# Expert slots into the dense layer: the last two slots' rows enter the first token block through products, and its gathers start two slots earlier

## Chip, cores and metric

One core of a Trainium2 chip (trn2) runs the whole program. The metric is the device time of one execution in microseconds.

## What is computed

Three layers in a row: attention in which a query sees only keys of its own hash bucket (2 x 8 heads, 768 positions, 64 wide), a mixture of 8 experts with the best two per token, and a dense layer with a rational activation. The change touches the seam between the second and the third:

```python
top2 = np.argpartition(-noisy_logits, 2, axis=1)[:, :2]
...
for e in range(E):
    for k in range(2):
        mask = top2[:, k] == e
        h = np.maximum(x[mask] @ w1[e], 0.0)
        out[mask] += top2_w[mask, k, None] * (h @ w2[e])
# then, with x = out (1536 x 512):
h = x @ w_in
P = a[0] + a[1] * h + a[2] * h2 + a[3] * h3
Q = 1.0 + np.abs(b[0]) * np.abs(h) + np.abs(b[1]) * h2
return (P / (Q + 1e-06)) @ w_out
```

## The kernel before

**Experts.** Tokens are scattered into rows sorted by expert, and these are cut into 31 slots (`SLOTS`) of 128 rows, numbered 0 to 30. TensorE runs, in the call for slot i: `turn_h(i-1)` (8 transposes of the 1024 hidden values, L1128), `up(i)` (24 products with w1, L1110) and `down(i-1)` (24 products with w2 into the bank `ps_o`, L1136). After slot 30's `up` come `turn_h(30)` and `down(30)`. Weights and activations are split into a high and a low part, so every product is three. ScalarE writes the high part of the turned hidden values (L846), VectorE the low part (`split_h`, L1499), and `down` waits for that. VectorE copies a finished slot to `y_sb` (`copy_y`, L1505) and ScalarE's queue stores it to the table `y_slots` in DRAM (`store_y`, L854). In the call for slot i this is the store of slot i-2, issued behind `relu(i)`; the stores of slots 29 and 30 stand behind the loop.

**Seam.** A token's result is the weighted sum of two rows of `y_slots`. The dense layer takes the 1536 tokens in 4 blocks of 384 (`TB` = 3 tiles of 128). For the first block GpSimd waits until all 31 slots are stored (L689, L690) and issues six gathers (L693, two for each tile). ScalarE scales the first row of each token (L888), VectorE adds the second (`combine`, L1528), TensorE turns the sum (`turn_x2`, 4 transposes a tile, L1166), ScalarE and VectorE split it into high and low (L891, L1536), and `product_a` (L1169, 12 products with w_in) can begin.

**Dense layer.** For each of 16 columns of chunks f: `product_a(f)`, a chain of ScalarE, VectorE and GpSimd instructions for the activation (GpSimd's `product`, L704, is one of them), and `product_b(f)` (L1181, 9 products with w_out), which TensorE takes three steps later (`LAG`). `product_a(f)` waits for the activation of f-4.

**GpSimd's order** at the seam is that of its program: the splits of w_in; after `up(30)` two loads of w_out's first half into the high part (`cast_hi`, L577); the six gathers; the loads of the second half; the splits of chunks 0 to 3 of w_out (L569: low part = raw - high; each needs its high part and a raw chunk in a ring of two that SyncE fills when the chunk two before is split, L450); then `product(0, 0)`, then the gathers of the next block (L713) between the products. The second half of that weight buffer is read by `down(30)`, the first half by `up(30)`.

## Time and profile before

| what | us |
|---|---|
| time before, median of 3 runs | 983.32 (982.04 to 985.05) |
| profiled execution: its time | 980.57 |
| profiled execution: span | 978.7 |
| TensorE busy | 912.2 (93% of the span) |
| VectorE, ScalarE, GpSimd busy | 584.3, 495.7, 451.6 |

Matmuls are pipelined and their ends are modelled, so the time between two starts says more than the time of one. In the span, attention runs to about 288 us, routing to 306 us, the experts to 678 us and the dense layer to the end.

### The profile page before, as it was taken

Reading aid. Unit: us, or ns where it says so; the run is one execution under the profiler, and the core shown is the slowest. Engines: PE = TensorE matmul, PEld = TensorE weight load, DVE = VectorE, ACT = ScalarE, POOL = GpSimd, SP = SyncE. Lnnn points to the kernel's source line nnn. Section 1 sums busy time; section 2 is a strip of 40 time slices with the busy share of each in tenths; the row PEclk is TensorE's granted clock in tenths of the full one; section 3 lists DMA queues with packets and bytes.
Section 4 is the critical chain, followed back from the end, with each engine's and each line's share of the span. In section 5 each row is a group of like instructions: output and inputs, shape, how many; then the busy total and the mean of one; then the engine's idle time right before and its main releaser. Section 6 shows DMA issues by size and latency. Waiting matters only on the chain.

```text
span 978.7 us, 17801 instructions
## 1 busy us (share of the span) xinstructions
PE 912.2 (93%) x5505; PEld 787.2 (80%) x5506; DVE 584.3 (60%) x1232; ACT 495.7 (51%) x886; POOL 451.6 (46%) x361
## 2 busy tenths in 40 slices
PE   5899999999964999999999999996599999999998
PEld 5788888888853888888888888884489999999997
DVE  7689988899774322222222222221598878877775
ACT  3677787778641222222222222220477877777775
POOL 5633353335444545645644446501767554463221
PEclk9899999999996999999999999999799999999999
DMA  9963554253239768867958587814712100110000
GB/s 199 272 207 89 127 134 126 75 134 80 95 128 279 221 213 282 273 214 236 298 183 279 178 271 243 261 46 130 228 41 66 55 23 22 54 43 0 33 1 32
DMA packets 88148, 143.63 MB, mean 147 GB/s; under 512 B 15522, under 2 KB 47778, under 8 KB 87586
## 3 DMA queue, kind: packets, MB, share of 16 engines
q1 hardware_dynamic: 47026, 72.46, 25.1%
q0 software_dynamic: 19328, 54.53, 17.6%
q10 hardware_dynamic: 21744, 16.00, 5.8%
q8 instruction: 28, 0.46, 0.2%
q14 instruction: 22, 0.18, 0.1%
HBM read 123.30 MB, written 19.66 MB: 146 GB/s over the span
## 4 chain that ended last, share of the span: by engine, by line
PE 73%; DVE 10%; issue 4%; DMA 4%; POOL 3%; SPq 3%; ACT 2%; DVEq 0%; another core or an unknown queue 0%; ACTq 0%; POOLq 0%
PE ps_s L1122 18%; PE ps_o L1147 17%; PE ps_s L1190 13%; PE ps_t L1176 6%; DVE mx L1281 4%; PE ps_s L1176 4%; PE ps_m L1176 3%; PE ps_s L1133 3%; PE ps_o L1017 2%; PE ps_t L1004 2%; DMA q_in<-in_q 2%; PE ps_s L995 1%; DVE qm L1271 1%; DMA k_in<-in_k 1%; SPq L439 1%
## 5 line engine op out<-in xcount | busy, mean ns | idle before, releaser
L569 POOL TENSOR_TENSOR w_r<-raw,w_r 128x1024 f32 (+1 forms) x72 | 171.9, 2402 | 107.8 <-DMA raw<-in_moe_w 46.3
L1122 PE MATMUL ps_s<-w_r,xT 128*128 x744 | 178.7, 396 | 14.4 <-DVE xT L1495 14.4
L1147 PE MATMUL ps_o<-w_r,hT 128*128 x744 | 174.0, 389 | 2.6 <-DVE hT L1499 2.6
L1122 PEld LDWEIGHTS ps_s<-w_r,xT 128*128 128x128 f32 x744 | 138.6, 190 | 42.4 <-issue 14.6
L1147 PEld LDWEIGHTS ps_o<-w_r,hT 128*128 128x128 f32 x744 | 139.6, 188 | 31.7 <-issue 2.8
L1190 PE MATMUL ps_s<-w_r,g_r 128*128 128x512 f32 x576 | 145.3, 397 | 4.6 <-DVE g_r L1581 4.6
L1505 DVE COPY y_sb<-ps_o 128x512 f32<-128x512 f32 x31 | 21.4, 691 | 209.9 <-PE ps_o L1147 209.9
L1190 PEld LDWEIGHTS ps_s<-w_r,g_r 128*128 128x128 f32 x576 | 107.5, 189 | 25.2 <-issue 4.5
L704 POOL TENSOR_TENSOR m<-q,g_r 128x384 f32<-128x384 f32 x64 | 65.6, 1024 | 113.8 <-DVE g_r L1569 113.6
L846 ACT ACTIVATE hT<-ps_s 128x1024 fp32r<-128x1024 f32 x31 | 31.8, 1026 | 160.2 <-DVE y_sb L1505 111.1
L763 ACT ACTIVATE prob<-ps_s,nb,sc 128x768 f32<-128x768 f32 x96 | 95.1, 991 | 19.7 <-DVE nb L1286 19.0
L756 ACT ACTIVATE probT<-ps_t 128x768 f32<-128x768 f32 x93 | 75.3, 810 | 40.5 <-PE ps_t L1004 40.5
L1281 DVE TENSOR_REDUCE mx<-ps_s 128x1 f32<-128x768 f32 x96 | 91.3, 951 | 2.7 <-PE ps_s L996 1.4
L1004 PE MATMUL ps_t<-ident,prob 128*128 128x128 f32 x570 | 81.8, 280 | 1.3 <-ACT probT L756 1.0
L995 PE MATMUL ps_s<-km,qm 128*128 128x512 f32 x192 | 71.3, 374 | 3.7 <-ACT prob L763 2.6
L1017 PE MATMUL ps_o<-probT,v_in 128*64 128x128 f32 x1128 | 72.0, 277 | 1.8 <-DVE x_sb L1305 1.8
L1176 PE MATMUL ps_t<-x2T,w_r 128*128 (+1 forms) x384 | 72.3, 337 | 0.0
L1004 PEld LDWEIGHTS ps_t<-ident,prob 128*128 128x128 f32 x570 | 63.1, 142 | 9.8 <-issue 9.8
L1547 DVE SCALAR_TENSOR_TENSOR v<-s,ab,t 128x384 f32<-128x384 f32 x64 | 47.8, 747 | 38.1 <-ACT t L902 37.9
L609 POOL TENSOR_TENSOR qs<-tile_t,qs 64x768 fp32r<-64x768 f32 x14 | 25.4, 1818 | 97.3 <-ACT qs L795 97.2
L1176 PEld LDWEIGHTS ps_t<-x2T,w_r 128*128 128x128 f32 x384 | 68.2, 188 | 2.6
L1017 PEld LDWEIGHTS ps_o<-probT,v_in 128*64 128x64 f32 x1128 | 60.7, 137 | 9.6 <-issue 9.5
(240 smaller groups left out, 1481.7 us busy)
## 6 DMA issues: line engine op xcount, KB each, us to landing
w_r<-in_moe_w POOLq DMA_DIRECT2D x32, 1024.0 KB, 8.5
raw<-in_moe_w SPq DMA_DIRECT2D x56, 512.0 KB, 4.1
q_in<-in_q SPq DMA_DIRECT2D x56, 176.0 KB, 3.5
k_in<-in_k SPq DMA_DIRECT2D x56, 176.0 KB, 4.3
y_slots<-y_sb ACTq DMA_DIRECT2D x31, 256.0 KB, 4.4
xg<-x_slots ACTq DMA_DIRECT2D x120, 64.0 KB, 3.7
raw<-in_moe_w SPq DMA_DIRECT2D x16, 256.0 KB, 2.8
raw<-in_moe_w_in SPq DMA_DIRECT2D x8, 512.0 KB, 5.7
```

The costliest lines, as they stand in the source:

```text
L569: pool.tensor_tensor(of_chunk(buf, 1, n), raw[:, par, :], of_chunk(buf, 0, n).bitcast(F), ALU.subtract).then_inc(split_done, 1)
L704: pool.tensor_tensor(m2[:], q2[:, f % 2, :], g_r[:, f % 4, 0, :].bitcast(F), ALU.mult).then_inc(m_ready, 1)
L756: act.activation(probT[:, hh, t % 2, :], src[:, 0:S], ACT.Copy).then_inc(pt_ready[hh], 1)
L763: act.activation(prob[:, hh, t % 2, :], ps_s[hh][:, 0:S], ACT.Exp, bias=nb[:, i:i + 1], scale=sc[:, i:i + 1], accum_out=rs[:, hh, t:t + 1] ...
L995: pe.matmul(o, qm[:, par, hh, rows], km[:, par, hh, c0:c1], start=True, stop=False)
L1004: mm = pe.transpose(to[:, u * P:(u + 1) * P], prob[:, hh, t % 2, u * P:(u + 1) * P], ident[:])
L1017: mm = pe.matmul(to[64 * hh:64 * hh + 64, 0:P], v_in[:, par, hh, u * D:(u + 1) * D], probT[:, hh, t % 2, u * P:(u + 1) * P], start=(u == 0 ...
L1122: mm = pe.matmul(ps_s[0][:, o * 512:o * 512 + 512], xT[:, par, part, c * P:c * P + P], w_r[:, buf, wpart, col:col + 512], start=(c == 0 an ...
L1147: mm = pe.matmul(ps_o[:, :], hT[:, part, c * P:c * P + P], w_r[:, buf, wpart, col:col + DM], start=(c == 0 and part == 0 and wpart == 0), ...
L1176: mm = pe.matmul(ps_a[f % 4], w_r[:, 0, wpart, c * FF2 + f * P:c * FF2 + f * P + P], x2T[:, par, part, c, :], start=(c == 0 and wpart == 0 ...
L1190: mm = pe.matmul(ps_b[j], g_r[:, f % 4, part, j * P:j * P + P], w_r[:, 1, wpart, f * DM:f * DM + DM], start=(f == 0 and part == 0 and wpar ...
L1281: dve.tensor_reduce(mx[:, i:i + 1], ps_s[hh][:, 0:S], AX.X, ALU.max).then_inc(row_max_done[hh], 1)
```

## The change

- `y_slots` counts as sure up to slot 28 (`SURE` = 29 x 128 rows). The gathers of the first block read only that part, at positions cut off at `SURE - 1`, and wait for the stores up to slot 28. The weights `w_sure` are 0 for a token whose row lies beyond.
- What slots 29 and 30 owe to the 384 tokens is a matrix of weights: `late_w`, made by VectorE after its first two `split_x` (six comparisons with a row of numbers from GpSimd, one sum), turned by TensorE in the call for slot 2 (6 transposes) and copied to `late_T` by ScalarE.
- `first_sum` takes the place of `turn_x2` for the first block: 4 products of a tile's sum with the identity, 4 with slot 29's rows and weights, 4 with slot 30's, all added up in one bank, for three tiles: 36 f32 products for 12 transposes.
- In the call for slot 30 TensorE puts `turn_h(30)` in the middle of `down(29)`; slot 30 has its own `hT_last` and writes another bank.
- VectorE does the three `combine` before it copies slots 29 and 30; ScalarE scales before it stores them.
- GpSimd issues the gathers first, then the loads of w_out's first half, its four splits, and the loads of the second half.

```diff
+LATE = 2
+SURE = (SLOTS - LATE) * P
...
-    y_pos_i = small("y_pos_i", [P, 2, NT], U32)
+    y_sure = small("y_sure", [P, 2, TB], F)
+    y_sure_i = small("y_sure_i", [P, 2, TB], U32)
+    w_sure = small("w_sure", [P, 2, TB], F)
...
+    hT_last = at("hT_last", 148 * KB, [P, 2, FF], R)
+    late_w = at("late_w", 136 * KB, [P, TB, LATE * P], F)
+    late_b = at("late_b", 139 * KB, [P, TB, LATE * P], F)
+    late_row = at("late_row", 142 * KB, [P, LATE * P], F)
+    late_T = at("late_T", 193 * KB, [P, TB, LATE, P], F)
...
-    y_first = at("y_first", c[0] - 12 * KB, [P, TB, 2, DM], F)
+    y_first = at("y_first", 156 * KB, [P, TB, 2, DM], F)
...
-    x2_first = at("x2_first", c[0] - 6 * KB, [P, TB, DM], F)
+    x2_first = at("x2_first", 168 * KB, [P, TB, DM], F)
...
-    x2_bank = [ps_o[:, :], ps_t[:, 0:512], ps_t[:, 512:1024]]
+    first_bank = [ps_t[:, 0:512], ps_t[:, 512:1024], ps_m[:, :]]
+    late_bank = ps_t[:, 0:TB * LATE * P]
...
+    def last_slot(i):
+        return isinstance(i, int) and i == SLOTS - 1
+    def hT_of(i):
+        return hT_last if last_slot(i) else hT
+    def y_bank(i):
+        return ps_s[0][:, 0:512] if last_slot(i) else ps_o[:, :]
...
+            pool.wait_ge(lg_ready, 1 + len(GROUPS))
+            pool.iota(late_row[:], [[1, LATE * P]], base=SURE, channel_multiplier=0,
+                      allow_small_or_imprecise_dtypes=True).then_inc(late_row_set, 1)
...
+            pool.wait_ge(sure_ready, 1)
+            pool.wait_ge(y_stored[0], 16 * ((SLOTS - LATE + 1) // 2))
+            pool.wait_ge(y_stored[1], 16 * ((SLOTS - LATE) // 2))
+            for j in range(TB):
+                for kk in range(2):
+                    pool.indirect_dma_start(y_first[:, j, kk, :], None, y_slots[0:SURE, :],
+                                            bass.IndirectOffsetOnAxis(ap=y_sure_i[:, kk, j:j + 1], axis=0)).then_inc(y_first_got[j][kk], 16)
             pool.wait_ge(h_ready, SLOTS + 1)
             cast_hi(1, wout_h[0], DM, 0)
-            pool.wait_ge(y_pos_ready, 1)
-            pool.wait_ge(y_stored[0], 16 * ((SLOTS + 1) // 2))
-            pool.wait_ge(y_stored[1], 16 * (SLOTS // 2))
-            for j in range(TB):
-                for kk in range(2):
-                    pool.indirect_dma_start(y_first[:, j, kk, :], None, y_slots,
-                                            bass.IndirectOffsetOnAxis(ap=y_pos_i[:, kk, j:j + 1], axis=0)).then_inc(y_first_got[j][kk], 16)
+            split_some(E + 1, 1, range(CHUNKS // 2))
+            pool.wait_ge(slot_done, SLOTS + 1)
             cast_hi(1, wout_h[1], DM, CHUNKS // 2)
-            split_some(E + 1, 1, range(4))
...
             def gather_y(n, i, j, kk):
                 if kk == 0:
...
+                    if isinstance(n, int) and n == 0 and j == 0:
+                        pool.wait_ge(y_stored[0], 16 * ((SLOTS + 1) // 2))
+                        pool.wait_ge(y_stored[1], 16 * (SLOTS // 2))
...
                 relu(i)
+                if isinstance(i, int) and i == 2:
+                    act.wait_ge(late_turned, 1)
+                    act.activation(late_T[:].rearrange("p j s t -> p (j s t)"), late_bank, ACT.Copy).then_inc(late_ready, 1)
...
             slots(act, act_slot)
             hT_hi_out(SLOTS - 1)
-            for i in (SLOTS - 2, SLOTS - 1):
-                store_y(i, i % 2)
-            act.wait_ge(weights_ready, 1)
+            act.wait_ge(sure_ready, 1)
...
-                act.activation(ps_b[j], y_first[:, j, 0, :], ACT.Copy, scale=wts[:, 0, j:j + 1]).then_inc(y_scaled, 1)
+                act.activation(x2_first[:, j, :], y_first[:, j, 0, :], ACT.Copy, scale=w_sure[:, 0, j:j + 1]).then_inc(y_scaled, 1)
+            for i in (SLOTS - 2, SLOTS - 1):
+                store_y(i, i % 2)
...
-                act.activation(x2T[:, 0, 0, :, j * P:j * P + P], x2_bank[j].rearrange("p (c t) -> p c t", c=DC),
+                act.activation(x2T[:, 0, 0, :, j * P:j * P + P], first_bank[j].rearrange("p (c t) -> p c t", c=DC),
...
-            def down(i):
+            def down(i, part=range(FC)):
...
+                if part[0] == 0:
+                    pe.wait_ge(split_done, e * CHUNKS + CHUNKS)
+                    pe.wait_ge(hT_ready, i + 1)
+                    if not last_slot(i) and (not isinstance(i, int) or i > 0):
+                        pe.wait_ge(y_ready, i)
+                for c in part:
+                    for half, whalf in ((0, 0), (0, 1), (1, 0)):
...
+                        mm = pe.matmul(y_bank(i), hT_of(i)[:, half, c * P:c * P + P], w_r[:, buf, whalf, col:col + DM],
...
+                if part[-1] == FC - 1:
+                    mm.then_inc(slot_done, 1)
+            def turn_late():
+                pe.wait_ge(late_made, 2 * TB + 1)
+                for j in range(TB):
+                    for s in range(LATE):
+                        mm = pe.transpose(late_bank[:, (j * LATE + s) * P:(j * LATE + s + 1) * P], late_w[:, j, s * P:s * P + P], ident[:])
+                mm.then_inc(late_turned, 1)
...
             def pe_slot(i, half, par, y, nxt):
...
-                down(i - 1)
+                if isinstance(i, int) and i == 2:
+                    turn_late()
+                if last_slot(i):
+                    down(i - 1, range(0, FC // 2))
+                    turn_h(i)
+                    down(i - 1, range(FC // 2, FC))
+                else:
+                    down(i - 1)
             slots(pe, pe_slot)
-            turn_h(SLOTS - 1)
...
+            def first_sum(j, slot):
+                if slot is None:
+                    pe.wait_ge(x2_ready, j + 1)
+                for c in range(DC):
+                    cols = slice(c * P, c * P + P)
+                    if slot is None:
+                        mm = pe.matmul(first_bank[j][:, cols], x2_first[:, j, cols], ident[:],
+                                       start=(c == 0), stop=False, skip_group_check=True)
+                    else:
+                        mm = pe.matmul(first_bank[j][:, cols], y_sb[:, slot % 2, cols], late_T[:, j, slot - SLOTS + LATE, :],
+                                       start=False, stop=(slot == SLOTS - 1 and c == DC - 1), skip_group_check=True)
+                return mm
+            pe.wait_ge(late_ready, 1)
...
-                pe.wait_ge(x2_ready, j + 1)
-                turn_x2(x2_first[:, j], x2_bank[j])
+                first_sum(j, None)
+            for slot in range(SLOTS - LATE, SLOTS):
+                pe.wait_ge(y_ready, slot + 1)
+                for j in range(TB):
+                    mm = first_sum(j, slot)
+                    if slot == SLOTS - 1:
+                        mm.then_inc(x2_turned, 1)
...
-            dve.tensor_copy(y_pos_i[:], y_pos[:]).then_inc(y_pos_ready, 1)
+            link(dve.tensor_scalar(y_sure[:], y_pos[:, :, 0:TB], float(SURE - 1), None, ALU.min))
...
-            dve.tensor_tensor(wts[:, 1, :], wts[:, 1, :], wts[:, 0, :], ALU.mult).then_inc(weights_ready, 1)
+            link(dve.tensor_tensor(wts[:, 1, :], wts[:, 1, :], wts[:, 0, :], ALU.mult),
+                 dve.tensor_copy(y_sure_i[:], y_sure[:]))
+            dve.scalar_tensor_tensor(out=w_sure[:], in0=y_pos[:, :, 0:TB], scalar=float(SURE), in1=wts[:, :, 0:TB],
+                                     op0=ALU.is_lt, op1=ALU.mult).then_inc(sure_ready, 1)
...
+            dve.wait_ge(late_row_set, 1)
+            for j in range(TB):
+                for kk, to in ((0, late_w), (1, late_b)):
+                    dve.tensor_scalar(to[:, j, :], late_row[:], y_pos[:, kk, j:j + 1], wts[:, kk, j:j + 1],
+                                      ALU.is_equal, ALU.mult).then_inc(late_made, 1)
+            dve.wait_ge(late_made, 2 * TB)
+            dve.tensor_tensor(late_w[:], late_w[:], late_b[:], ALU.add).then_inc(late_made, 1)
+            def combine(j):
+                dve.wait_ge(y_scaled, j + 1)
+                dve.wait_ge(y_first_got[j][1], 16)
+                dve.scalar_tensor_tensor(out=x2_first[:, j, :], in0=y_first[:, j, 1, :], scalar=w_sure[:, 1, j:j + 1],
+                                         in1=x2_first[:, j, :], op0=ALU.mult, op1=ALU.add).then_inc(x2_ready, 1)
             def dve_slot(i, half, par, y, nxt):
...
-                copy_y(i - 1, (i - 1) // 2, 1 - par)
+                if not last_slot(i):
+                    copy_y(i - 1, (i - 1) // 2, 1 - par)
             slots(dve, dve_slot)
             split_h(SLOTS - 1)
+            for j in range(TB):
+                combine(j)
+            copy_y(SLOTS - 2, (SLOTS - 2) // 2, (SLOTS - 2) % 2)
             copy_y(SLOTS - 1, (SLOTS - 1) // 2, (SLOTS - 1) % 2)
-            def combine(j):
-                y = y_first[:, j]
-                dve.wait_ge(y_scaled, j + 1)
-                dve.wait_ge(y_first_got[j][1], 16)
-                dve.scalar_tensor_tensor(out=x2_first[:, j, :], in0=y[:, 1, :], scalar=wts[:, 1, j:j + 1],
-                                         in1=ps_b[j], op0=ALU.mult, op1=ALU.add).then_inc(x2_ready, 1)
...
-                split_x2(0, 0, j, x2_bank[j])
+                split_x2(0, 0, j, first_bank[j])
+            dve.wait_ge(y_stored[0], 16 * ((SLOTS + 1) // 2))
+            dve.wait_ge(y_stored[1], 16 * (SLOTS // 2))
```

GpSimd at the seam, as the two programs have it. Before:

```order
L569 TENSOR_TENSOR w_r<-raw,w_r 128x1024 x6
L577 DMA w_r<-in_moe_w_out 128x4x512 x2
L693 DMA y_first<-y_slots,y_pos_i 128x512 x6
L577 DMA w_r<-in_moe_w_out 128x4x512 x2
L569 TENSOR_TENSOR w_r<-raw,w_r 128x1024 x4
L704 TENSOR_TENSOR m_145<-q_141,g_r 128x384
```

After:

```order
L592 TENSOR_TENSOR w_r<-raw,w_r 128x1024 x6
L717 DMA y_first<-y_slots,y_sure_i 128x512 x6
L600 DMA w_r<-in_moe_w_out 128x4x512 x2
L592 TENSOR_TENSOR w_r<-raw,w_r 128x1024 x4
L600 DMA w_r<-in_moe_w_out 128x4x512 x2
L731 TENSOR_TENSOR m_152<-q_148,g_r 128x384
```

The six gathers moved ahead of the first two loads, and the last two loads behind the four splits, just ahead of the first `product`. VectorE from the low part of slot 29's turned values on, now:

```order
L1570 TENSOR_TENSOR hT<-ps_s,hT 128x1024
L1570 TENSOR_TENSOR hT_last<-ps_s,hT_last 128x1024
L1594 SCALAR_TENSOR_TENSOR x_first<-y_first,w_sure,x_first 128x512 x3
L1576 COPY y_sb<-ps_o 128x512
L1576 COPY y_sb<-ps_s 128x512
L1618 TENSOR_TENSOR x2T<-ps_t,x2T 128x4x128 x2
L1618 TENSOR_TENSOR x2T<-ps_m,x2T 128x4x128
```

Both copies of late slots stand behind the three `combine`, which wait for the gathers.

## Rows read from the trace of the kernel before

**Rows 1.** Stages: busy us (instructions) of PE, PEld, DVE, ACT, POOL; PEclk; DMA share; GB/s

```profile
320.00:640.00 320.00, 320.00 (x1522) 267.00 (x1521) 88.18 (x109) 71.75 (x82) 170.10 (x104) 1.00 0.76 241
...
680.00:700.00 20.00, 7.74 (x28) 6.57 (x29) 4.30 (x7) 4.10 (x8) 12.10 (x10) 0.57 0.78 241
700.00:720.00 20.00, 15.81 (x78) 14.37 (x77) 18.03 (x26) 13.87 (x29) 14.65 (x12) 0.91 0.27 86
```

**Rows 2.** Chain that ended last, around slot 30's end: start, us, what

```profile
678.38 0.70 DVE y_sb L1505
...
679.11 2.02 DMA y_slots<-y_sb
```

**Rows 3.** Timeline of PE at the seam: start, us, instruction, [idle before <- releaser]

```profile
663.56 5.61 PE L1147 MATMUL ps_o<-w_r,hT 128*128 x24
669.01 1.03 PE L1133 MATMUL ps_s<-ident,h_sb 128*128 128x128 f32 x8
672.63 5.72 PE L1147 MATMUL ps_o<-w_r,hT 128*128 x24 [2.58 <-DVE hT L1499]
...
692.99 1.12 PE L1166 MATMUL ps_t<-ident,x_first 128*128 128x128 f32 x4 [1.65 <-DVE x_first L1528]
695.61 3.95 PE L1176 MATMUL ps_s<-x2T,w_r 128*128 128x384 f32 x12 [1.50 <-POOL w_r L569]
699.40 2.27 PE L1176 MATMUL ps_m<-x2T,w_r 128*128 128x384 f32 x12
701.51 4.33 PE L1176 MATMUL ps_t<-x2T,w_r 128*128 128x384 f32 x24
710.03 3.61 PE L1190 MATMUL ps_s<-w_r,g_r 128*128 128x512 f32 x9 [4.19 <-DVE g_r L1581]
```

**Rows 4.** Timeline of ScalarE's queue: the store of slot 28

```profile
663.77 0.34 ACTq L854 DMA_DIRECT2D y_slots<-y_sb  x1
```

**Rows 5.** Timeline of POOL at the seam

```profile
681.98 1.03 POOL L693 DMA_INDIRECT y_first<-y_slots,y_pos_i  x1 [16.41 <-DMA y_slots<-y_sb]
...
688.35 0.95 POOL L693 DMA_INDIRECT y_first<-y_slots,y_pos_i  x1 [0.30 <-issue]
689.30 1.62 POOL L577 DMA_DIRECT2D w_r<-in_moe_w_out  x2
690.90 4.70 POOL L569 TENSOR_TENSOR w_r<-raw,w_r 128x1024 fp32r<-128x1024 f32 x2
700.47 5.08 POOL L569 TENSOR_TENSOR w_r<-raw,w_r 128x1024 fp32r<-128x1024 f32 x2 [4.87 <-DMA raw<-in_moe_w_out]
705.72 0.99 POOL L704 TENSOR_TENSOR m<-q,g_r 128x384 f32<-128x384 f32 x1 [0.18 <-DVE g_r L1569]
```

**Rows 6.** Timeline of DVE at the seam

```profile
692.19 0.75 DVE L1528 SCALAR_TENSOR_TENSOR x_first<-y_first,wts,ps_s 128x512 f32<-128x512 f32 x1 [2.01 <-DMA y_first<-y_slots,y_pos_i]
...
700.66 2.62 DVE L1547 SCALAR_TENSOR_TENSOR v<-s,ab,t 128x384 f32<-128x384 f32 x1 [5.02 <-ACT t L902]
```

**Rows 7.** Timeline where the experts begin

```profile
304.27 0.73 DVE L1491 STREAM_TRANSPOSE ps_m<-xg 128x512 f32<-128x512 f32 x1 [1.91 <-DMA xg<-x_slots]
...
305.80 3.01 POOL L577 DMA_DIRECT2D w_r<-in_moe_w  x4 [7.06 <-DMA xg<-x_slots]
...
317.59 1.22 DVE L1499 TENSOR_TENSOR hT<-ps_s,hT 128x1024 fp32r<-128x1024 f32 x1 [8.64 <-ACT hT L846]
```

**Rows 8.** DMA issues around the seam: KB each, us to landing

```profile
w_r<-in_moe_w_out POOLq DMA_DIRECT2D x1, 1024.0 KB, 6.1
...
raw<-in_moe_w_out SPq DMA_DIRECT2D x6, 512.0 KB, 3.7
```

**Rows 9.** The six gathers L693; then POOL's weight loads L577, 540 to 700 us

```profile
DMA to landing us min/median/max: 3.3/3.5/3.8
...
DMA to landing us min/median/max: 5.7/8.5/12.9
```

**Rows 10.** Timeline of PE in attention: one f32 product (x2), then the next product

```profile
149.98 0.48 PE L1029 MATMUL ps_o<-turn_w,oT 128*128 x2
...
150.22 0.49 PE L995 MATMUL ps_s<-km,qm 128*128 128x512 f32 x1
```

More of the change, by code:

```diff
@@ L1134, in turn_h @@
                 mm.then_inc(h_turned, 1)
-            def down(i):
+            def down(i, part=range(FC)):
                 e = expert_of(i)
                 buf = e % 2
-                pe.wait_ge(split_done, e * CHUNKS + CHUNKS)
-                pe.wait_ge(hT_ready, i + 1)
-                if not isinstance(i, int) or i > 0:
-                    pe.wait_ge(y_ready, i)
-                for c in range(FC):
-                    for part, wpart in ((0, 0), (0, 1), (1, 0)):
-                        col = WCOLS + c * DM
-                        mm = pe.matmul(ps_o[:, :], hT[:, part, c * P:c * P + P], w_r[:, buf, wpart, col:col + DM],
-                                       start=(c == 0 and part == 0 and wpart == 0),
-                                       stop=(c == FC - 1 and part == 1))
-                mm.then_inc(slot_done, 1)
+                if part[0] == 0:
[5 more added lines that the diff above has]
+                    for half, whalf in ((0, 0), (0, 1), (1, 0)):
+                        col = WCOLS + c * DM
+                        mm = pe.matmul(y_bank(i), hT_of(i)[:, half, c * P:c * P + P], w_r[:, buf, whalf, col:col + DM],
+                                       start=(c == 0 and half == 0 and whalf == 0),
+                                       stop=(c == FC - 1 and half == 1))
+                if part[-1] == FC - 1:
[6 more added lines that the diff above has]
+                mm.then_inc(late_turned, 1)
             up(0, 0)
@@ L1538, in _ @@
             for j in range(TB):
-                combine(j)
-            for j in range(TB):
-                split_x2(0, 0, j, x2_bank[j])
+                split_x2(0, 0, j, first_bank[j])
+            dve.wait_ge(y_stored[0], 16 * ((SLOTS + 1) // 2))
+            dve.wait_ge(y_stored[1], 16 * (SLOTS // 2))
             dve.wait_ge(ab_ready, 1)
```

18 lines of the change are left out of this document (11 added, 7 removed).

## The prediction

> **What bounds the kernel now.** I read the stages first, then the chain of waits, then each engine's timeline at the seam. Among the experts TensorE is busy all 320 of 320 us at the full clock [rows 1]: what takes TensorE time away there, or adds to it, moves the end by as much. From 680 to 700 us it is busy 7.74 of 20 us, at a granted clock of 0.57. That hole is what the change aims at. In the chain, slot 30's last product ends at 678.38, where the copy begins, and the store lands at 679.11 + 2.02 = 681.13 [rows 2]. GpSimd begins the first gather 0.85 us later, at 681.98, and the sixth at 688.35 [rows 5]; the last `combine` starts at 692.19 [rows 6], the last four transposes at 692.99, and `product_a(0)` at 695.61 [rows 3]. So 17.2 us lie between the end of `down(30)` and the dense layer's first product. Before that, TensorE idles 2.58 us for the low part of slot 30's turned values [rows 3]. After it come four `product_a`, then 4.19 us idle until the first activation is there, and `product_b(0,0)` starts at 710.03 [rows 3]. The releaser printed at 695.61, GpSimd's split, is only the nearest event: the code waits there for the splits of w_in, long done, and for the split of the turned tiles. From 710 us on TensorE is nearly without a gap, so what this start gains the end gains.
>
> **The start of the experts: nothing, and 0.7 us.** VectorE's extra work in routing is two or three instructions on 6 columns ahead of the transpose at 304.27, which waits 1.91 us for its data; the six comparisons and the sum stand in the 8.64 us before 317.59 [rows 7]. Neither kind of 256 columns has a row; seven at the 0.75 us of the 512-column sum [rows 6] would be 5.3 us, still inside. GpSimd's row of numbers stands in the 7.06 us before 305.80 [rows 7]. Without these covers they would cost their own length, a few us at most. ScalarE's copy of 768 columns lies in a slot of which it uses a fraction (71.75 of 320 us [rows 1]). TensorE has no such cover: 8 transposes take 1.03 us with a tail [rows 3], some 0.11 us each, so six cost **+0.7 us**, and everything below is shifted by that.
>
> **TensorE to the end of `down(30)`.** `up(30)` ended where `down(29)` starts to run in earnest, 663.7 [rows 3], and now ends near 664.4. `down(29)` with `turn_h(30)` in its middle takes 5.45 + 0.9 us (starts of rows 3: 663.56 to 669.01, and 8 x 0.11), to 670.8. The second half of `down(29)`, 2.7 us, lies beside the two instructions for which TensorE waited 2.58 us, so that wait goes. `down(30)` then ends at 670.8 + 5.7 = 676.5.
>
> **Gathers.** The store of slot 28 is issued at 663.77 [rows 4], now 664.4, and lands after 2.0 us. With the same 0.85 us to the first gather, that begins at 667.3, and the sixth 6.37 us later (681.98 to 688.35 [rows 5]), at 673.7. It lands 3.8 us after [rows 9], at 677.5, and `combine` of the last tile takes 0.75 [rows 6]: 678.2. TensorE by then has done the eight products of the first two tiles (1.8 us from 676.5). So the gathers are no longer ahead of the end alone; the two chains meet, and the gathers end last by a little.
>
> **The products.** An f32 product is two records: 160 columns took 0.24 us to the next start [rows 10]. Below it cannot fall under two of the 0.11 us of a transpose. I take 0.23. VectorE copies slots 29 and 30 after the last `combine`, by 679.6, hidden behind TensorE: four products of the third tile (0.9) to 679.2 and 24 (5.5) to 684.7. From the last turning to `product_a(0)` it was 695.61 - 694.11 = 1.5 us [rows 3]; the same now gives **686.2 against 695.61, -9.4 us**. The lower bound for a product, one record of 0.11 us, would give 28 x 0.12 = 3.4 us more; the upper bound is a rival below.
>
> **The clock.** `product_a(0)` took 3.79 us to the next start, the second 2.11 [rows 3]: the first ran at the 1.2 GHz level after the long idle time. Now TensorE works nearly without a hole up to 684.7 and should keep the 2.4 GHz level: **-1.7 us**. The idle time before `product_b(0,0)`, and the slow start after it, stay.
>
> **GpSimd must keep up.** It issues the loads of w_out's first half at 674.6 instead of 664.03. The first landed after 6.1 us [rows 8]; I give it 1 us for the gathers still under way: 681.7. Two splits take 4.7 us [rows 5], to 686.4. The raw chunks for the next two are asked for at 684.1 and 686.4 and take 3.7 us each [rows 8], so the third split runs from 687.8, the fourth from 690.2 to 692.6. The two loads of the second half take 1.6 us [rows 5]: 694.2. `product(0,0)` was due 6.3 us after `product_a(0)` gave way to the next (699.40 to 705.72 [rows 3, 5]), now at 688.3 + 6.3 = 694.6. GpSimd is there 0.4 us early: cost 0. VectorE's first instruction of the activation, 2.62 us beside a running split [rows 6], stays as long, since a split still runs beside it. The gathers of the next block now queue behind 2 MB of weight loads; the steps after the first have slack, and I give them 0 to 2 us in the range.
>
> **Sum.** +0.7 is contained in the times above; -9.4 - 1.7 = -11.1 us. The profiled execution took 980.57 us (span 978.7), which gives 969.5; it lies 2.75 us under the median, and from the median the forecast is 983.3 - 11.1 = **972.2 us**. Its own range: with products at the lower bound 968.8, and 968.5 with some spread of the median; next block's gathers late by 2 us, 974.5.
>
> **The rivals.**
> 1. *GpSimd becomes the wait (0.15).* Its weight loads took 5.7 to 12.9 us to land [rows 9]. At 12.9 instead of 7.1 the splits end 5.8 us later, all but 0.4 on the path: 972.2 + 5.4 = 977.6. For it: the order now puts splits, loads and `product(0,0)` in a row with hardly a margin. Against: the long landings fell beside other loads, and the DMA engines are free here.
> 2. *A product costs four transposes (0.08).* By rows 3 and 10 it costs about two. If it were 4 x 0.11 = 0.44 us, the 28 products after 678.2 would take 28 x 0.21 = 5.9 us more: 978.1. The Trainium skill says this ("TensorE: Matmul & The Clock Gate", Terms: the transpose mode is 4 times faster for FP32) and so speaks against giving up transposes; the measured start-to-start of 0.24 us speaks against the factor here.
> 3. *The clock falls during the products (0.06).* If TensorE is granted the 1.2 GHz level from 678 us on, 28 products take 6.4 us more and `product_a(0)` keeps its 1.7: 980.3. For it: before, the clock fell at this place. Against: then TensorE had nothing from 678.38 until the first gather landed, past 681.98 + 3.3 = 685.3 [rows 2, 5, 9]; now the hole is under 1 us.
> 4. *Slower (0.04): the copies of slots 29 and 30 stuck behind late gathers.* VectorE does them after the last `combine`. If a gather landed like the slowest load, 12.9 us after 673.7, `combine` would end at 687.3; TensorE would idle from 678 and fall to 1.2 GHz: 28 products of 0.46 us to 700.2, 1.5 us, `product_a(0)` at 701.7 with the slow clock, 6.1 us later than before: 989.4. It decides from a `combine` end of about 681, with the slow clock. Against: six gathers all landed within 3.8 us [rows 9], and now without weight loads ahead.
> 5. *The store of slot 28 doesn't free the gathers early, or the gain is given back at the first activation (0.03): 983.* Against it: the semaphore counts in the code, and no other engine than those above has work there.
>
> **Chances.** The forecast has 0.64. 0.3% of the time, 3 us, is about what a measurement of this kernel tells from no change. Forecast, 1 and 2 are faster by more: 0.87, and I add 0.01 of rival 3; 3 and 5 are within it: 0.08; slower 0.04. The range that leaves out 3, 4, 5 and the odd end is 968.5 to 978.5.
>
> **What the profile after would show.** `down(30)` with no idle time before it; the first gather near 667 and the last `combine` near 678; 36 f32 products (72 records) that end near 685; `product_a(0)` near 686 with about 2.1 us to the next; `product(0,0)` near 694.5 released by VectorE and not by a DMA; `product_b(0,0)` near 698.6. The prediction is wrong if the wait before GpSimd's splits or before the third `combine` is long, if the spacing of the products is not near 0.23 us, or if the granted clock between 676 and 695 is below 0.9.

## The result, and the profile after

| what | us |
|---|---|
| time after, median of 6 runs | 971.98 (969.77 to 973.55) |
| time before beside it, median of 6 runs | 983.02 (982.01 to 985.82) |
| ratio | 0.9887, 95% interval 0.9871 to 0.9903 |
| profiled execution after: span | 970.7 |

The change takes 11.0 us off (9.5 to 12.7 by the interval). The forecast was 11.1 us off, to 972.2 us.

The busy times of the page after show no work gone; TensorE has 3.4 us more than the 912.2 before, VectorE 2.3.

```profile
PE 915.6 (94%) x5571; PEld 790.9 (81%) x5572; DVE 586.6 (60%) x1241; ACT 496.6 (51%) x887; POOL 452.8 (47%) x362
```

The stages after (us busy of PE, PEld, DVE, ACT, POOL with their instructions; PEclk; DMA share; GB/s), against [rows 1]:

```profile
320.00:640.00 320.00, 320.00 (x1524) 267.09 (x1523) 88.28 (x109) 72.72 (x83) 171.13 (x105) 1.00 0.76 242
680.00:700.00 20.00, 16.05 (x113) 15.37 (x111) 9.99 (x15) 8.09 (x17) 12.95 (x9) 1.00 0.75 243
700.00:720.00 20.00, 18.41 (x83) 16.25 (x84) 16.95 (x28) 12.98 (x27) 12.07 (x13) 0.91 0.45 139
```

The hole is what went: 16.05 us busy at a granted clock of 1.00, where it was 7.74 at 0.57. The timeline of PE after at the seam, against [rows 3]:

```profile
667.06 2.89 PE L1180 MATMUL ps_o<-w_r,hT 128*128 x12
669.79 1.03 PE L1165 MATMUL ps_s<-ident,h_sb 128*128 128x128 f32 x8
670.58 2.98 PE L1180 MATMUL ps_o<-w_r,hT 128*128 x12
673.45 5.73 PE L1180 MATMUL ps_s<-w_r,hT_last 128*128 x24
679.02 1.95 PE L1253 MATMUL ps_t<-ident,x_first 128*128 128x128 f32 x16
681.56 1.16 PE L1253 MATMUL ps_m<-ident,x_first 128*128 128x128 f32 x8 [0.60 <-DVE x_first L1594]
...
687.02 1.06 PE L1256 MATMUL ps_m<-late_T,y_sb 128*128 128x128 f32 x8
689.59 2.32 PE L1224 MATMUL ps_s<-x2T,w_r 128*128 128x384 f32 x12 [1.50 <-DVE x2T L1618]
691.74 2.24 PE L1224 MATMUL ps_m<-x2T,w_r 128*128 128x384 f32 x12
...
701.57 3.73 PE L1238 MATMUL ps_s<-w_r,g_r 128*128 128x512 f32 x9 [3.42 <-DVE g_r L1663]
```

`down(29)` (L1180), `turn_h(30)` (L1165), the rest of `down(29)` and `down(30)` follow each other with no idle time; the first idle time is 0.60 us, for the third `combine`. Then 36 products (72 records) run, and `product_a(0)` (L1224) has the full clock, 2.15 us to the next.

GpSimd after, against [rows 5]:

```profile
670.14 1.03 POOL L717 DMA_INDIRECT y_first<-y_slots,y_sure_i  x1 [31.86 <-DMA y_slots<-y_sb]
...
676.84 0.94 POOL L717 DMA_INDIRECT y_first<-y_slots,y_sure_i  x1 [0.30 <-issue]
677.79 1.63 POOL L600 DMA_DIRECT2D w_r<-in_moe_w_out  x2
685.40 4.66 POOL L592 TENSOR_TENSOR w_r<-raw,w_r 128x1024 fp32r<-128x1024 f32 x2 [5.98 <-DMA w_r<-in_moe_w_out]
691.54 5.07 POOL L592 TENSOR_TENSOR w_r<-raw,w_r 128x1024 fp32r<-128x1024 f32 x2 [1.48 <-DMA raw<-in_moe_w_out]
696.57 1.54 POOL L600 DMA_DIRECT2D w_r<-in_moe_w_out  x2
698.11 1.02 POOL L731 TENSOR_TENSOR m<-q,g_r 128x384 f32<-128x384 f32 x1
```

`product(0,0)` (L731) starts without idle time right behind GpSimd's own loads: it wasn't VectorE that it waited for. The chain that ended last says the same: behind the sixth gather it runs through GpSimd and its transfers up to `product(0,0)`, then through VectorE to `product_b(0,0)`, and TensorE's 36 products aren't in it:

```profile
677.79 7.53 DMA w_r<-in_moe_w_out
...
685.40 2.36 POOL w_r L592
...
687.77 3.64 DMA raw<-in_moe_w_out
```

The last `combine` and the first activation on VectorE, against [rows 6]:

```profile
680.76 0.75 DVE L1594 SCALAR_TENSOR_TENSOR x_first<-y_first,w_sure,x_first 128x512 f32<-128x512 f32 x1 [2.13 <-DMA y_first<-y_slots,y_sure_i]
...
693.00 1.35 DVE L1629 SCALAR_TENSOR_TENSOR v<-s,ab,t 128x384 f32<-128x384 f32 x1 [2.56 <-ACT t L934]
```

The six gathers landed in 3.8 us each:

```profile
DMA to landing us min/median/max: 3.8/3.8/3.8
```

**How the traces are compared.** Two executions of one kernel begin the experts at different times: the first `up` starts at 309.25, 303.64 and 306.20 us in three traces of the changed kernel, at 306.65 in the one of the kernel before. That spread lies ahead of the seam, and 2.6 us of it (309.25 against 306.65) are why the two profiled spans differ by only 8.0 us. From the first `up` to the end the three traces of the change take 661.45, 662.86 and 663.00 us, the one of before 672.05: 9.1 to 10.6 us less. At the seam I count from the start of `down(29)`. All columns are us from the PE timelines: to `product_a(0)`, from there to `product_b(0,0)`, their sum, and from there to the end of the span.

| kernel | to a(0) | a(0) to b(0,0) | to b(0,0) | b(0,0) to end |
|---|---|---|---|---|
| before | 32.05 | 14.42 | 46.47 | 268.67 |
| after | 22.53 | 11.98 | 34.51 | 269.13 |
| after_again | 22.48 | 12.25 | 34.73 | 269.95 |
| after_beside | 21.85 | 13.63 | 35.48 | 269.57 |
| middle_alone | 29.20 | 14.23 | 43.43 | 268.98 |
| gathers_late | 35.03 | 11.21 | 46.24 | 268.95 |
| no_middle | 25.90 | 10.81 | 36.71 | 267.39 |
| late_first | 21.65 | 13.08 | 34.73 | 269.89 |
| loads_first | 27.26 | 10.82 | 38.08 | 268.90 |
| psum_scaled | 22.04 | 12.09 | 34.13 | 269.73 |
| loads_psum | 22.87 | 10.80 | 33.67 | 268.93 |
| turn_early | 22.40 | 11.95 | 34.35 | 269.74 |
| all_four | 21.66 | 10.80 | 32.46 | 268.91 |
| all_four_again | 21.66 | 10.81 | 32.47 | 267.41 |

Two things make up nearly all of the last column's spread. `product_b(0,0)` and the `product_a` behind it take 5.5 to 5.8 us to the next start in eleven of the fourteen traces, but 4.3 in no_middle and all_four_again and 4.6 in psum_scaled, where they had a higher clock (last section). And the second and third `product_b` wait up to 1.9 us together where the next block's gathers land late.

### The profile page after: what moved, and what is told of

Read it like the earlier page. It is cut to its first block, busy times and chain, and to the rows that moved or that the text cites. A ratio compares the mean times of both kernels' runs of the same rounds, so it can differ in the third digit from the quotient of the medians.

```text
span 970.7 us, 17952 instructions
## 1 busy us (share of the span) xinstructions
PE 915.6 (94%) x5571; PEld 790.9 (81%) x5572; DVE 586.6 (60%) x1241; ACT 496.6 (51%) x887; POOL 452.8 (47%) x362
## 4 chain that ended last, share of the span: by engine, by line
PE 72%; DVE 9%; DMA 6%; issue 5%; POOL 3%; SPq 3%; ACT 2%; DVEq 0%; ACTq 0%; POOLq 0%
PE ps_s L1154 18%; PE ps_o L1180 16%; PE ps_s L1238 14%; PE ps_t L1224 7%; DVE mx L1349 4%; PE ps_s L1224 3%; PE ps_m L1224 3%; PE ps_s L1165 3%; PE ps_o L1049 2%; DMA q_in<-in_q 2%; PE ps_t L1036 2%; SPq L462 1%; DMA k_in<-in_k 1%; PE ps_s L1027 1%; DVE tile_t L1326 1%
## 5 line engine op out<-in xcount | busy, mean ns | idle before, releaser
L1180 PE MATMUL ps_o<-w_r,hT 128*128 x720 | 168.6, 390 | 0.0
L1180 PEld LDWEIGHTS ps_o<-w_r,hT 128*128 128x128 f32 x720 | 135.0, 188 | 27.9
L731 POOL TENSOR_TENSOR m<-q,g_r 128x384 f32<-128x384 f32 x64 | 66.0, 1031 | 110.9 <-DVE g_r L1651 110.5
L1224 PE MATMUL ps_t<-x2T,w_r 128*128 (+1 forms) x384 | 72.4, 337 | 0.0
L1224 PEld LDWEIGHTS ps_t<-x2T,w_r 128*128 128x128 f32 x384 | 68.2, 188 | 2.6
```

The source lines that it names most:

```text
L731: pool.tensor_tensor(m2[:], q2[:, f % 2, :], g_r[:, f % 4, 0, :].bitcast(F), ALU.mult).then_inc(m_ready, 1)
L1180: mm = pe.matmul(y_bank(i), hT_of(i)[:, half, c * P:c * P + P], w_r[:, buf, whalf, col:col + DM], start=(c == 0 and half == 0 and whalf == 0),
L1224: mm = pe.matmul(ps_a[f % 4], w_r[:, 0, wpart, c * FF2 + f * P:c * FF2 + f * P + P], x2T[:, par, part, c, :], start=(c == 0 and wpart == 0 ...
```

## The experiments

Three groups of kernels were measured, each on one chip beside the kernel before. The first has after_again, gathers_late, no_middle and loads_first (median of before 979.57 us), the second middle_alone, late_first, loads_psum and all_four (982.03), the third after_beside, psum_scaled, turn_early and all_four_again (984.05). Ratios are to the kernel before of the same group, intervals at 95%; the second group has no run of the change beside it, so its kernels are compared with the change by their ratios. Theory: the early gathers carry the gain, the middle of `down(29)` a small part, and GpSimd is just in time. The rival I took most seriously was that GpSimd's loads and splits have become the wait.

**after_again, after_beside: the changed kernel again.**

> The changed kernel once more, as the measure for the runs beside it. All theories: about 0.989 of the kernel before, 972 us. It also shows whether the experts' late start (309.25 us in the profile after, 306.65 before) belongs to the change: if the new instructions at routing delay it, it starts 2 us or more later than in before's profile here too; if it is spread of the attention stage and its transfers, the start moves by as much either way.

> The changed kernel beside the three others on the same chip: 0.9886 of the kernel before (0.987 to 0.990).

Measured: 968.3 us, ratio 0.9883 (0.9860 to 0.9905), and 971.3 us, 0.9878 (0.9860 to 0.9896). The gain is the same on both.

**gathers_late: the gathers wait for slot 30's products too.**

```diff
             pool.wait_ge(sure_ready, 1)
+            pool.wait_ge(slot_done, SLOTS + 1)
```

> The change with the gathers made to wait for the end of down(30) too (but not for its store): the suspected wait doubled. The first gather starts at about 680 instead of 670.1, 9.7 us later. Theory that the gathers' issue and landing end last: the third combine ends 9.7 us later and product_a(0) at least 9.1 us later; with TensorE idle for some 9 us its clock falls, 28 products take 0.43 us each instead of 0.22, and that costs up to 6 us more and 1.7 us in product_a(0): 9 to 16 us slower than the change, so as slow as before or slower. Rival, the gain came from the missing store and from the copies, with the early gathers worth little: under 4 us slower.

Measured: 980.6 us, ratio 1.0005 (0.9991 to 1.0020): all of the gain is gone. The PE timeline, and the window around it with a granted clock of 0.62:

```profile
683.24 2.05 PE L1254 MATMUL ps_t<-ident,x_first 128*128 128x128 f32 x8 [6.62 <-DVE x_first L1595]
...
689.43 2.08 PE L1254 MATMUL ps_m<-ident,x_first 128*128 128x128 f32 x8 [1.27 <-DVE x_first L1595]
691.30 3.17 PE L1257 MATMUL ps_t<-late_T,y_sb 128*128 128x128 f32 x16
```

```profile
678.00:696.00 18.00, 10.70 (x56) 10.14 (x57) 3.45 (x5) 2.16 (x3) 11.34 (x10) 0.62 0.80 237
```

`product_b(0,0)` comes 46.24 us after `down(29)` began, 11.7 later than in the change, for gathers that begin 9.9 us later (at 677.48, 12.97 after `down(29)`, against 3.08). The starts divide the 11.7. The third tile's products begin 10.4 us later (24.92 us after `down(29)` against 14.50). They and the first 8 of slot 29's products, at the lower clock, take 1.87 and 3.00 us to the next start against 1.00 and 1.79: 2.1 more. And 0.8 comes back before `product_b(0,0)`, since here GpSimd was done first and waited 1.38 us for VectorE. The edit holds back GpSimd's loads too (they stand behind the gathers), which by this wait cost nothing at the seam. Everything else of the change is still in this kernel, so with late gathers the products, the saved wait of `down(30)` and GpSimd's new order are together worth nothing, though the first gather still begins 5.4 us sooner after `down(29)` than in the kernel before (12.97 against 18.42).

**middle_alone: the kernel before with `turn_h(30)` in the middle of `down(29)`** (and with `hT_last` and the other bank, which this needs).

```diff
                 up(i, par)
-                down(i - 1)
...
+                if last_slot(i):
+                    down(i - 1, range(0, FC // 2))
+                    turn_h(i)
+                    down(i - 1, range(FC // 2, FC))
+                else:
+                    down(i - 1)
```

> The kernel before with one part of the change alone: turn_h(30) in the middle of down(29), with hT_last and the other bank; gathers, transposes and GpSimd's order as before. Theory: everything behind down(30) is a chain in that kernel, so the wait of 2.58 us is saved whole: 2.6 us faster than the kernel before, ratio 0.9974. Rival, the gain is lost at the loads of w_out's first half, which are then still under way when slot 30 is stored: under 1 us.

Measured: 978.05 us (975.19 to 980.37), ratio 0.9951 (0.9932 to 0.9969): 3.0 to 6.7 us. Its trace gives 3.0 us at `product_b(0,0)`: `down(30)` has no idle time before it, and the long waits stand where they stood:

```profile
672.48 5.73 PE L1158 MATMUL ps_s<-w_r,hT_last 128*128 x24
687.48 1.11 PE L1182 MATMUL ps_o<-ident,x_first 128*128 128x128 f32 x4 [9.27 <-DVE x_first L1546]
```

The 2.6 us expected lie outside the interval by little. The trace is at its edge, and it is of the slowest of the seven runs (980.37 us, the fastest took 975.19), so the 1.0 us between it and the median's 4.0 isn't explained. With gathers_late this divides the 12.0 us of the seam: 3.0 for the middle (46.47 to 43.43), 2.8 back for what else gathers_late has, above all, as I read it, the products that there lie in the open in place of transposes (to 46.24), and 11.7 for the early gathers (to 34.51). Another order of the steps would divide it otherwise.

**no_middle: the change without the middle.** The edit is the one above, reversed.

> The change without turn_h(30) in the middle of down(29): TensorE waits again for the low part, 2.6 us. Theory that the gathers end last: the third combine is ready 0.6 us after the first eight products, so only 2.6 - 0.6 = 2.0 us reach product_a(0), and since product(0,0) waits for GpSimd's splits and not for TensorE alone, 0.5 to 1 us less reach product_b(0,0): 1 to 1.5 us slower than the change. Rival, TensorE alone sets the end of the seam: all 2.6 us. Rival, GpSimd's chain alone sets it: nothing.

Measured: 969.44 us (967.84 to 969.95), ratio 0.9893 (0.9872 to 0.9915), 1.1 us above the change beside it, which the intervals don't tell from nothing. The PE timeline and the window from 671 to 674:

```profile
670.91 7.24 PE L1180 MATMUL ps_s<-w_r,hT_last 128*128 x24 [2.63 <-DVE hT_last L1566]
```

```profile
671.00:674.00 3.00, 3.00 (x7) 2.39 (x8) 1.01 (x2) 1.11 (x2) 2.56 (x3) 0.50 0.72 216
```

`down(30)` waited 2.63 us and then took 7.1 us to the next start where it takes 5.6, since the granted clock was 0.50. So `product_a(0)` was 3.4 us later, more than the 2.6 of the wait. But 1.4 came back before `product_b(0,0)`: GpSimd, whose chain doesn't depend on this, was done first and waited for VectorE:

```profile
694.20 1.00 POOL L731 TENSOR_TENSOR m<-q,g_r 128x384 f32<-128x384 f32 x1 [3.05 <-DVE g_r L1647]
```

This is the first sign that the change's own order leaves GpSimd late: 10.81 us from `product_a(0)` to `product_b(0,0)` against 12 to 13.6 in three traces of the change. At `product_b(0,0)` the trace is 2.0 us behind the one of after_again, and behind that it is 2.6 ahead (267.39 against 269.95): 1.5 by the higher clock there, 0.75 since the third `product_b` doesn't wait. So the median's 1.1 is no measure of what the middle is worth at the seam, and that it lies in the expected range is in part luck.

**late_first: TensorE takes slot 29's 12 products before the gathered tiles, VectorE copies slot 29 before the three `combine`.** This takes away the wait for the third tile.

```diff
+            copy_y(SLOTS - 2, (SLOTS - 2) // 2, (SLOTS - 2) % 2)
             for j in range(TB):
                 combine(j)
-            copy_y(SLOTS - 2, (SLOTS - 2) // 2, (SLOTS - 2) % 2)
```

> The change with another order of the same 36 products and of VectorE's copies: slot 29 is copied before the combines and its 12 products come first, then the 12 of the gathered tiles, then slot 30's 12. Theory that TensorE's wait of 0.55 to 0.6 us for the third combine is the only hole between down(30) and the last product: that hole and the start of each group behind a wait go, product_a(0) is 0.6 to 1.0 us earlier; but the first product on GpSimd waits for the splits (chain of waits after), so product_b(0,0) and the end gain at most 0.3 us. Rival, TensorE sets the end: all of 0.6 to 1.0 us.

Measured: 971.27 us (970.48 to 971.79), ratio 0.9886 (0.9866 to 0.9907): no difference from the change's 0.9887. `product_a(0)` came at 21.65 us, 0.2 to 0.9 sooner, and `product_b(0,0)` at 34.73, no sooner. GpSimd again went to L731 with no idle time:

```profile
694.80 1.54 POOL L600 DMA_DIRECT2D w_r<-in_moe_w_out  x2
696.34 1.02 POOL L731 TENSOR_TENSOR m<-q,g_r 128x384 f32<-128x384 f32 x1
```

So TensorE's part of the seam can become shorter without the end coming sooner: GpSimd's loads and splits are the wait.

**loads_first: GpSimd loads w_out's first half ahead of the gathers**, as before the change.

```diff
+            pool.wait_ge(h_ready, SLOTS + 1)
+            cast_hi(1, wout_h[0], DM, 0)
             pool.wait_ge(sure_ready, 1)
...
-            pool.wait_ge(h_ready, SLOTS + 1)
-            cast_hi(1, wout_h[0], DM, 0)
             split_some(E + 1, 1, range(CHUNKS // 2))
```

> The change with the two loads of w_out's first half ahead of the gathers again, as before. Theory that GpSimd's chain (loads, splits, loads, product) has become the wait: the splits end about 8 us earlier, product(0,0) is released by VectorE, and 0.5 us or more are gained, if the six gathers land as late as now (the loads, 5.5 us of data, are through by 675 and the last gather is issued at 676.8). Rival, contention: the gathers land behind the 2 MB, and the splits run beside the combines on the shared path of VectorE; the third combine ends 2 to 3 us later and the kernel is 1.5 to 2.5 us slower.

Measured: 970.33 us (969.28 to 972.02), ratio 0.9901 (0.9879 to 0.9922), 2.0 us slower than the change beside it. The intervals overlap, but only one of the change's six runs (969.50) is above the fastest of these. GpSimd was now early by far: it was idle for 10.81 us before `product(0,0)`. The rival had named what took the gain, the splits beside the three `combine`, and its 1.5 to 2.5 us. GpSimd's timeline, VectorE's, and the durations in the view of the tile `x_first`:

```profile
673.57 4.69 POOL L592 TENSOR_TENSOR w_r<-raw,w_r 128x1024 fp32r<-128x1024 f32 x2
679.39 2.36 POOL L592 TENSOR_TENSOR w_r<-raw,w_r 128x1024 fp32r<-128x1024 f32 x1 [1.14 <-DMA raw<-in_moe_w_out]
...
696.88 1.01 POOL L731 TENSOR_TENSOR m<-q,g_r 128x384 f32<-128x384 f32 x1 [10.81 <-DVE g_r L1651]
```

```profile
674.46 7.84 DVE L1594 SCALAR_TENSOR_TENSOR x_first<-y_first,w_sure,x_first 128x512 f32<-128x512 f32 x3 [5.25 <-ACT x_first L918]
```

```profile
L1594 DVE SCALAR_TENSOR_TENSOR x_first<-y_first,w_sure,x_first x3: 739/2897/4360, 674.5 to 679.4; 128x512 f32<-128x512 f32 x3
```

The first `combine` took 4.36 us, from 674.46 to 678.82, and ended 0.56 us behind the second split (678.26). The second took 0.74 and fell nearly whole into the pause between the splits. The third took 2.90, from 679.4 to 682.3, and ended 0.55 us behind the third split (681.75). So a `combine` that met a split ended only when the split had. The other half of the rival is there too, but smaller: the gathers landed after 4.3 to 7.4 us where the change has 3.8, and ScalarE had scaled the third row at 677.0, 1.1 us later after `down(29)` than in the change, while the third `combine` ended 4.7 later. TensorE waited 3.71 us and then had a lower clock:

```profile
678.96 3.43 PE L1253 MATMUL ps_t<-ident,x_first 128*128 128x128 f32 x16 [3.71 <-DVE x_first L1594]
```

**psum_scaled and loads_psum: the scaled rows in PSUM banks.** In the kernel before, `combine` read one operand from PSUM; the change made it two from SBUF. Both kernels let ScalarE write the scaled rows to PSUM banks (two of the three parts held slot 30's turned values, so it first waits until VectorE has read them); loads_psum has the order of loads_first as well. With the change and loads_first these are all four pairs of bank and order.

```diff
+    scaled = [ps_s[0][:, 512:1024], ps_s[1][:, 0:512], ps_s[1][:, 512:1024]]
...
-                act.activation(x2_first[:, j, :], y_first[:, j, 0, :], ACT.Copy, scale=w_sure[:, 0, j:j + 1]).then_inc(y_scaled, 1)
+                if j == 1:
+                    act.wait_ge(hT_ready, SLOTS)
+                act.activation(scaled[j], y_first[:, j, 0, :], ACT.Copy, scale=w_sure[:, 0, j:j + 1]).then_inc(y_scaled, 1)
```

> The loads of w_out's first half ahead of the gathers, as in loads_first, and ScalarE's scaled rows put in PSUM instead of SBUF, so that the combines have one SBUF input. Theory that loads_first lost its time to the sharing between VectorE and GpSimd (three combines over 7.84 us beside the splits, with two SBUF inputs each): the combines take 0.75 us again, product_a(0) comes 22.5 to 23 us after the start of down(29) instead of 27.3, and GpSimd is early for its first product: 0.5 to 1.5 us faster than the change. Rival, the combines are late since the gathers land behind the loads: product_a(0) stays 26 us or more after it and the time stays 2 us over the change.

> Edit against the change: ScalarE writes the scaled first rows of the three tiles into PSUM banks and not into SBUF, so each combine reads one operand from SBUF; the order of GpSimd's work is the change's own. Theory A (the bank matters only because GpSimd's splits then run beside the combines, which they do not in the change's order, where the combines took 0.75 us): no difference, 0.9885 of the kernel before, within 0.0015. Theory B (the bank makes the combine itself or the release of the products earlier, and the loads' order did little): as the version with both, 0.9865.

Measured: loads_psum 968.92 us (967.50 to 970.29), ratio 0.9864 (0.9842 to 0.9886), 2.3 us below late_first beside it (all four runs below all four of late_first); psum_scaled 972.49 us (971.25 to 974.29), ratio 0.9891 (0.9873 to 0.9909). That is 1.2 us above the change beside it, but the intervals overlap and from `down(29)` to the end its trace is 1.2 us shorter, so no difference is shown. So the banks are worth something only where a split runs beside the `combine`. In loads_psum one does (GpSimd), and the `combine` keep their 0.75 us (tile `x_first`):

```profile
674.90 4.71 POOL L593 TENSOR_TENSOR w_r<-raw,w_r 128x1024 fp32r<-128x1024 f32 x2
...
693.85 1.00 POOL L732 TENSOR_TENSOR m<-q,g_r 128x384 f32<-128x384 f32 x1 [5.86 <-DVE g_r L1654]
```

```profile
L1597 DVE SCALAR_TENSOR_TENSOR x_first<-y_first,w_sure,ps_s x3: 747/748/748, 676.0 to 678.5; 128x512 f32<-128x512 f32 x3
```

And GpSimd is idle for 5.86 us before `product(0,0)`: it is the wait no more, and `product_a(0)` to `product_b(0,0)` is 10.80 us. The 1.2 to 2.8 us by which GpSimd was late in the change are recovered. Of the 2.3 us against late_first the traces show 1.1 up to `product_b(0,0)` (34.73 to 33.67) and 1.0 behind it, 0.74 of which is the third `product_b`'s wait for the next block's gathers: these no longer queue behind the last two loads, which GpSimd now issues at 686.38, ahead of `product_a(0)`.

**turn_early: the six transposes of the late weights behind `up(0)`.**

```diff
             up(0, 0)
+            turn_late()
...
-                if isinstance(i, int) and i == 2:
-                    turn_late()
```

> Edit against the change: the six transposes of the late weights stand right behind up(0), where TensorE waits for the turned slot 1, and not behind up(2), where nothing was idle. Theory: 0.57 us less, since the wait covers them: 0.9880 of the kernel before where the change has 0.9886; within 5 rounds this is hardly told from no difference. Rival: the comparisons that make the weights end after the wait does, so that TensorE waits for them and the start of up(1) is later by up to 3 us: 0.990 to 0.992. The start of up(1) in the timeline tells the two apart.

Measured: 972.98 us (971.93 to 973.67), ratio 0.9891 (0.9872 to 0.9909), 1.7 us above the change beside it with overlapping intervals: no gain is seen. The rival fell: the transposes stand without idle time behind `up(0)` and inside the wait for ScalarE,

```profile
317.57 0.82 PE L1191 MATMUL ps_t<-ident,late_w 128*128 128x128 f32 x6
318.85 1.09 PE L1165 MATMUL ps_s<-ident,h_sb 128*128 128x128 f32 x8 [0.46 <-ACT h_sb L880]
```

and from the first `turn_h` to `down(29)` it takes 348.56 us against 349.21, 349.17 and 349.27 in the three traces of the change: 0.6 to 0.7 us are saved there. But its experts began at 310.53, the latest of all. That the saving reaches the end isn't shown; it is below what the medians tell.

**all_four, all_four_again: loads_psum, late_first and turn_early together.**

> The change with four edits: loads of w_out's first half ahead of the gathers, scaled rows in PSUM, slot 29's products first, and the six transposes of the weights right behind up(0), where TensorE waits 1.11 us for ScalarE. Theory: the transposes' 0.6 us go, product_a(0) comes 0.6 to 1 us earlier than in the change, and nothing is lost at GpSimd: 2 to 3 us faster than the change, ratio to before about 0.986. Rival, as in loads_psum: slower than the change.

> The version with all four edits a second time, beside the change on the same chip: 0.9850 of the kernel before and 3 to 4 us below the change. If the earlier 0.9847 was the chip's or the day's spread, it comes out at 0.987 or above, within 2 us of the change.

Measured: 967.31 us (965.38 to 969.91), ratio 0.9847 (0.9825 to 0.9868), and 966.55 us (964.74 to 969.33), ratio 0.9829 (0.9807 to 0.9851), beside 971.30 us, 0.9878, for the change: 4.7 us below it, with intervals that don't touch. `product_b(0,0)` stands at 32.46 and 32.47 us. With GpSimd out of the way, late_first's earlier products now count: 1.2 us sooner than loads_psum, of which late_first alone gave nothing. Of the 4.7 us the traces show 3.0 at `product_b(0,0)` (35.48 to 32.47), 0.65 in a third `product_b` that no longer waits, and 0.6 to 0.7 from the transposes. That trace has 1.4 more by the higher clock at `product_b(0,0)`, which all_four, the same kernel, doesn't have.

## Why the prediction was right

Its steps were laid out as times of one trace; here they are from the start of `down(29)` (664.26 in the prediction: 663.56 and the 0.7 of `turn_late`).

| step | predicted | measured, first trace after |
|---|---|---|
| first gather | 3.0 | 3.08 |
| sixth gather | 9.4 | 9.78 |
| end of the last `combine` | 13.9 | 14.45 |
| `product_a(0)` | 21.9 | 22.53 |
| first split of w_out | 17.4 | 18.34 |
| end of the fourth split | 28.3 | 29.55 |
| `product(0,0)` on GpSimd | 30.3 | 31.05 |
| `product_b(0,0)` | 34.3 | 34.51 |

- **turn_late, +0.7:** 0.57 us (336.26 to the next start at 336.83), 0.095 us for each transpose. The comparisons took 0.40 us each where 0.75 was the bound, and were hidden.
- **`down(30)` with no wait:** right, and alone worth 3.0 us at `product_b(0,0)` by middle_alone. In the change it is worth 3.4 us at `product_a(0)` but 2.0 at `product_b(0,0)` (no_middle), since GpSimd stands behind it. The prediction didn't see that.
- **The gathers:** the release by slot 28's store was right within 0.1 us. One of the six took 1.30 us to issue and not 0.95; that is the 0.35 that the sixth was late. gathers_late shows that the whole gain hangs on this step.
- **The products, 0.23 us:** slot 29's 12 take 2.68 us from start to start, 0.223 each, and a transpose 0.095 to 0.11. Two to two and a half transposes, then. Rival 2 is refuted: the factor of 4 that the Trainium skill ("TensorE: Matmul & The Clock Gate", Terms) gives for the transpose mode doesn't show in this kernel as a product at four times a transpose.
- **The clock, -1.7:** right; `product_a(0)` took 2.15 us and the granted clock was 1.00 from 680 to 700 us. Rival 3 did not occur.
- **GpSimd early by 0.4 us, cost 0: wrong.** This is the step that failed. It was late, in every trace of the change, by 1.2 to 2.8 us (12.0 to 13.6 us from `product_a(0)` to `product_b(0,0)`, where 10.8 is what is left when GpSimd waits for VectorE). Rival 1 named the mechanism, with a price of 5.4 us for loads that land in 12.9; the first load landed after 7.5 us (7.1 assumed), and each link was late by a few tenths. In after_beside, where the lateness is largest, the first split began 8.6 us behind the load's issue.
- **Why the total was right all the same:** a second term was wrong the other way. I left VectorE's first instruction of the activation at 2.62 us because a split would run beside it. One did, and it took 1.35; in loads_psum, with no split beside it, 0.62. What the rows show is a wait for the split's end, not a fixed length: before, the split ran from 700.47 to 702.87 and the instruction ended at 703.28; in the change the split ended at 693.94 and the instruction at 694.35, 0.41 us behind it both times. The prediction's 12.4 us from `product_a(0)` to `product_b(0,0)` was thus the right length made of the wrong pieces: a slow VectorE where it was a late GpSimd. That these two errors cancelled is luck: the forecast of 972.2 is closer to 971.98 than the reasoning deserved.
- **Two slips in the prediction's numbers.** The low end of the range takes a product at one record of 0.11 us, although the text has just said that it can't fall under two. And -11.1 us puts `product_b(0,0)` at 698.9, where the list of signs has 698.6; the table above goes by the list.
- **The next block's gathers, 0 to 2 us:** GpSimd waited 4.47 us at 707.28 for the first of them, and the third `product_b` was held up by 0 to 0.75 us in the traces of the change, 1.71 in psum_scaled. In range.
- **Rivals 4 and 5** did not occur. gathers_late ran into a weak form of rival 4: with the gathers late by 9.9 us it fell back to no gain, at a clock of 0.62, and not beyond.

## What to carry to other kernels

When the result of a serial chain (store, gather, sum) holds up a stage, bringing the last part of its input in as a product with a small matrix of weights lets the chain start earlier; here 9.9 us of earlier gathers were worth 11.7 at `product_b(0,0)`, the lower clock of the long wait included. It has its own price, which only the early start pays back: with late gathers the kernel was no faster than before. After such a change look at once for the engine that was hidden in the hole: here GpSimd, and a shorter TensorE path gave nothing until its loads were moved forward. Before work is moved beside another engine's, look at where both have their operands: the same reordering cost 2.0 us with two operands in SBUF and gained about 2.3 with one of them in PSUM (against late_first, which is as fast as the change).

## What was not expected of the hardware

- A VectorE `scalar_tensor_tensor` of 128x512 with two operands in SBUF took 4.36 and 2.90 us when it met GpSimd's splits of 2.35 us each, and 0.74 in the pause between them (loads_first); each of the two long ones ended 0.55 us behind the end of a split. With one operand in PSUM it took 0.75 us beside the same splits (loads_psum). The Trainium skill ("GPSIMD Engine Reference", Specifications) says that the SBUF interfaces are shared with VectorE, with contention for VectorE instructions with two SBUF inputs; these traces agree, and add the size.
- After an idle time of TensorE the granted clock fell in some cases and not in others. After 2.58 us in the kernel before, `down(30)` ran at 1.00 [rows 3]; after 2.63 us in no_middle at 0.50, the 1.2 GHz level. In all_four and all_four_again, the same kernel, `product_b(0,0)` came after 2.23 us idle both times and once took 3.83 us for its nine products and once 2.31 (granted clock from 697 to 703 us: 0.72 and 1.00); the rest of the span was 268.91 and 267.41 us. In psum_scaled it took 2.31 after a longer idle time, 3.50 us:

```profile
697.19 3.83 PE L1240 MATMUL ps_s<-w_r,g_r 128*128 128x512 f32 x9 [2.23 <-DVE g_r L1666]
```

```profile
697.49 2.31 PE L1240 MATMUL ps_s<-w_r,g_r 128*128 128x512 f32 x9 [2.23 <-DVE g_r L1666]
```

```profile
700.47 2.31 PE L1241 MATMUL ps_s<-w_r,g_r 128*128 128x512 f32 x9 [3.50 <-DVE g_r L1666]
```

  What decides it stays open. It is worth 1.5 us here, on top of the idle time itself, and it comes and goes between executions of one kernel, so a difference of that size between two traces says little.
- The experts of one and the same kernel began up to 5.6 us apart from one trace to the next. It goes in part with the group: 303.0 to 305.8 us in the traces of the first, 307.0 to 308.1 in the second, 306.2 to 310.5 in the third, and the medians of the kernel before rise in the same order. The cause, in attention or routing, wasn't looked for.
